# Attention in a fused kernel: where the transposes of the probabilities stand, and how the keys are cut

## What is computed

```python
def _attn_ref(q, k, v):                      # B, H, S, D = 2, 8, 1152, 64
    q_pool = q.reshape(B, H, S // 2, 2, D).mean(axis=3)
    scores = np.matmul(q_pool, k.transpose(0, 1, 3, 2)) / np.sqrt(D)
    scores = scores - np.max(scores, axis=-1, keepdims=True)
    attn = np.exp(scores)
    attn = attn / (np.sum(attn, axis=-1, keepdims=True) + 1e-09)
    return np.matmul(attn, v)

def reference(**kwargs):
    x = _attn_ref(q, k, v).transpose(0, 2, 1, 3).reshape(B * 576, 512)
    x = _moe_ref(x, ...)                     # sigmoid gate, 512 -> 1536 -> 512
    return _moe2_ref(x, ...)                 # 8 experts of width 1024, weights balanced in 8 rounds
```

## Time and profile before

| | us |
|---|---|
| median of 3 runs | 1244.61 (1244.44 to 1244.99) |
| the profiled execution | 1244.73 |
| its span on the core | 1242.9 |
| attention stage, from the start | about 262 |

### The profile page before, as it was taken

The page is one execution under the profiler, slowest core; times in us unless marked ns, Lnnn a source line. Parts: engine busy times, 40 slices in busy tenths (PEclk is TensorE's granted clock), DMA queues, the critical chain, the costliest instruction groups (busy, mean ns, idle before and its releaser), DMA issues.

```text
span 1242.9 us, 19939 instructions
## 1 busy us (share of the span) xinstructions
PE 1232.8 (99%) x7618; PEld 1130.9 (91%) x7618; DVE 798.2 (64%) x1682; ACT 594.6 (48%) x1239; POOL 631.9 (51%) x534
## 2 busy tenths in 40 slices
PE   8999999999999999999999999999999999999999
PEld 7888888899999899999998998998998998998998
DVE  7999999887873144776576376476466466466444
ACT  7999999854433344344353243243243233233221
POOL 6577777737873375654254254254254254254221
PEclk9999999999999999999999999999999999999999
DMA  6677767301112331221221222222222222222112
GB/s 172 120 114 126 120 120 120 87 26 34 52 35 68 111 94 52 68 86 51 69 73 64 69 75 62 68 72 65 67 70 68 68 69 69 64 73 68 52 34 93
DMA packets 98911, 95.37 MB, mean 77 GB/s; under 512 B 14528, under 2 KB 73152, under 8 KB 98816
## 3 DMA queue, kind: packets, MB, share of 16 engines
q1 hardware_dynamic: 98496, 93.77, 30.3%
q10 hardware_dynamic: 320, 0.33, 0.1%
HBM read 88.59 MB, written 2.40 MB: 73 GB/s over the span
## 4 chain that ended last, share of the span: by engine, by line
PE 92%; ACT 5%; DVE 1%; issue 1%; DMA 0%; ACTq 0%; POOL 0%; DVEq 0%; POOLq 0%
PE bank L1253 13%; PE bank L1255 13%; PE bank L1254 13%; PE bank L1506 11%; PE bank L1507 11%; PE bank L1508 11%; PE bank L1138 5%; PE bank L1111 4%; PE bank L1151 3%; PE bank L1152 3%; ACT probs L1615 2%; PE bank L1222 2%; PE bank L1220 2%; PE bank L1221 2%; ACT pT_hi L1534 2%
## 5 line engine op out<-in xcount | busy, mean ns | idle before, releaser
L2201 DVE TENSOR_TENSOR c<-bank,c 128x256 f32<-128x256 f32 (+1 forms) x448 | 197.3, 457 | 281.4 <-PE bank L1255 274.7
L1041 POOL TENSOR_TENSOR w_lo<-w_raw,w_hi 128x512 fp32r<-128x512 f32 x128 | 163.7, 1300 | 287.7 <-ACT w_hi L1534 287.7
L1507 PE MATMUL bank<-w_lo,h_hi 128*128 128x512 f32 x578 | 225.2, 390 | 0.0
L1506 PE MATMUL bank<-w_hi,h_hi 128*128 128x512 f32 x578 | 225.1, 390 | 0.0
L1508 PE MATMUL bank<-w_hi,h_lo 128*128 128x512 f32 x578 | 224.4, 388 | 0.0
L1814 ACT ACTIVATE h_hi<-c 128x256 fp32r<-128x256 f32 (+1 forms) x256 | 112.5, 445 | 160.3 <-DVE c L2201 160.0
L1508 PEld LDWEIGHTS bank<-w_hi,h_lo 128*128 128x128 f32 x578 | 108.5, 188 | 22.9
L1534 ACT ACTIVATE c<-bank 128x256 f32<-128x256 f32 (+1 forms) x64 | 26.2, 410 | 214.7 <-PE bank L1255 214.7
L1506 PEld LDWEIGHTS bank<-w_hi,h_hi 128*128 128x128 f32 x578 | 108.6, 188 | 20.8
L1970 DVE TENSOR_REDUCE part_min<-bank 128x1 f32<-128x256 f32 (+2 forms) x216 | 114.6, 558 | 20.0 <-PE bank L1152 13.7
L1507 PEld LDWEIGHTS bank<-w_lo,h_hi 128*128 128x128 f32 x578 | 108.6, 188 | 20.1
(11 more groups left out here) (206 smaller groups left out, 3142.9 us busy)
## 6 DMA issues: line engine op xcount, KB each, us to landing
w_raw<-in_moe_w SPq DMA_DIRECT2D x64, 512.0 KB, 3.6
w_raw<-in_moe_w SPq DMA_DIRECT2D x64, 256.0 KB, 3.1
q_raw<-in_q SPq DMA_DIRECT2D x30, 288.0 KB, 4.8
k_raw<-in_k SPq DMA_DIRECT2D x30, 288.0 KB, 7.6
wo_raw<-in_moe_w_out SPq DMA_DIRECT2D x16, 384.0 KB, 3.4
v_raw<-in_v SPq DMA_DIRECT2D x16, 288.0 KB, 4.9
gv_raw<-in_moe_w_gate SPq DMA_DIRECT2D x12, 256.0 KB, 2.9
gv_raw<-in_moe_w_val SPq DMA_DIRECT2D x12, 256.0 KB, 3.5
```

The lines of the kernel that those rows point to most:

```text
L1041: ins = nc.gpsimd.tensor_tensor(w2_lo[:, u % 2, c], w2_raw[:, c], f32(w2_hi[:, u % 2, c]), ALU.subtract)
L1506: nc.tensor.matmul(dst, hh, wh, start=(first and c == 0), stop=False)
L1507: nc.tensor.matmul(dst, hh, wl, start=False, stop=False)
L2201: nc.vector.tensor_tensor(dst[:, 0:w], bank[:, (u + b) % 3, 0:w], other[:, 0:w], ALU.add).then_inc(done, 1)
```

## The change

- The keys are cut into three parts of 384 (`KEYS`), at the start of banks 0, 1 and 2. The exponentials take parts 0 and 1 in one instruction of 768 keys, part 2 in one of 384. The pieces in which k is split become 768 and 384 (for the first head 384, 384 and 384).
- The reductions no longer write `part_min`. That of part 0 stores its least in bank 0's last column, next to part 1's first; the reduction of part 1 reads it with its scores and stores the result next to part 2; that of part 2 writes `nmax`. Parts 1 and 2 wait for the reduction before. The small reduction L1972 goes.
- On TensorE the transposes of g-1 stand behind the products with v. Their parts go round a ring of four banks (3, 6, 4, 5), and each waits for the `p_lo` of four parts before.
- ScalarE runs exponentials(g), the copies of outputs, `p_hi`(g-1, 0 to 2), and the splits of k and q. VectorE runs the reductions of g and then `p_lo`(g-2, 0 to 2).
- The common tile has no products with v any more; tiles 5 and 6 have nine instead of six, so that every tile but the common one has nine.

```diff
-KEYS = (0, 256, 640, 1152)
-SCORES_AT = (256, 512, 1024)
-EXP_KEYS = ((0, 640), (640, 1152))
-AV_STEPS = (9, 9, 9, 9, 6, 6, 6, 9, 9)
+KEYS = (0, 384, 768, 1152)
+EXP_PARTS = ((0, 2), (2, 3))
+FILL_RING = (3, 6, 4, 5)
+AV_STEPS = (9, 9, 9, 9, 0, 9, 9, 9, 9)
-KPIECES = ((0, 640), (640, 1152))
-FIRST_KPIECES = ((0, 256), (256, 640), (640, 1152))
+KPIECES = ((0, 768), (768, 1152))
+FIRST_KPIECES = ((0, 384), (384, 768), (768, 1152))
...
         def scores(j):
-            return columns[:, SCORES_AT[j]:SCORES_AT[j] + KEYS[j + 1] - KEYS[j]]
+            return bank[:, j, 0:KEYS[j + 1] - KEYS[j]]
+        def least(j):
+            return columns[:, 512 * j + 511:512 * j + 512]
+        def scores_and_least(j):
+            return columns[:, 512 * j - (j > 0):512 * j + KEYS[j + 1] - KEYS[j]]
         def fill_bank(g, j):
-            if j < 2:
-                return 3 + j
-            return 5 + g % 2 if g < PAIR * NHEAD // 2 - 1 else 5
+            return FILL_RING[(3 * g + j + (g == PAIR * NHEAD // 2 - 1)) % len(FILL_RING)]
...
 (TensorE, tile)
                 score(pair, i, 2)
-                if g >= 1:
-                    for j in range(NKB):
-                        if g >= 2 and j < 2:
-                            pe.wait_ge(p_lo_done, 3 * (g - 2) + j + 1)
-                        fill_p(g - 1, j)
                 if i < COMMON and pair >= 1:
                     ... av(2 * pair - 1, n)
                 if i >= COMMON:
                     ... av(2 * pair, n)
+                if g >= 1:
+                    for j in range(NKB):
+                        freed = 3 * (g - 1) + j - len(FILL_RING) + 1
+                        if freed > 0:
+                            pe.wait_ge(p_lo_done, freed)
+                        fill_p(g - 1, j)
...
 (ScalarE, tile)
-                for n, (k0, k1) in enumerate(EXP_KEYS):
-                    nc.scalar.activation(probs[g % 2][:, k0:k1],
-                                         columns[:, SCORES_AT[2 * n]:SCORES_AT[2 * n] + k1 - k0], ACT.Exp,
+                for n, (j0, j1) in enumerate(EXP_PARTS):
+                    k0, k1 = KEYS[j0], KEYS[j1]
+                    nc.scalar.activation(probs[g % 2][:, k0:k1].rearrange("p (j n) -> p j n", j=j1 - j0),
+                                         bank[:, j0:j1, 0:(k1 - k0) // (j1 - j0)], ACT.Exp,
...
+                outputs(pair, i)
                 if g >= 1:
-                    p_hi(g - 1, 2)
+                    for j in range(NKB):
+                        p_hi(g - 1, j)
                 between(pair, i)
-                p_hi(g, 0)
-                p_hi(g, 1)
...
 (VectorE, tile)
                 for j in range(NKB):
                     dve.wait_ge(s_ready, 3 * g + j + 1)
-                    nc.vector.tensor_reduce(part_min[:, t, j:j + 1], scores(j), AX.X, ALU.min).then_inc(min_done, 1)
-                dve.wait_ge(min_done, 3 * g + 3)
-                nc.vector.tensor_reduce(nmax[:, t:t + 1], part_min[:, t], AX.X, ALU.min).then_inc(nmax_done, 1)
-                if g >= 2:
-                    p_lo(g - 2, 2)
+                    if j >= 1:
+                        dve.wait_ge(min_done, 2 * g + j)
+                    last = j == NKB - 1
+                    nc.vector.tensor_reduce(nmax[:, t:t + 1] if last else least(j), scores_and_least(j), AX.X,
+                                            ALU.min).then_inc(nmax_done if last else min_done, 1)
                 if g < 2:
                     first_q_lo(g + 1)
+                else:
+                    p_lo(g - 2, 0)
+                    p_lo(g - 2, 1)
-                if g >= 1:
-                    p_lo(g - 1, 0)
                 ... reciprocals at i == 1 and i == 8
-                if g >= 1:
-                    p_lo(g - 1, 1)
+                if g >= 2:
+                    p_lo(g - 2, 2)
```

More of the change, by code:

```diff
@@ L164, in build @@
             o_all = allocate(s, [(f"o_all{n}", [PARTS, QLEN], F32) for n in range(ORING)])
-            o_other, r_rows, part_min, nmax, sums, den, rcol, split_scale = allocate(s, [
+            o_other, r_rows, nmax, sums, den, rcol, split_scale = allocate(s, [
                 ("o_other", [PARTS, QLEN], F32),
                 ("r_rows", [PARTS, QLEN], F32),
-                ("part_min", [PARTS, QT, NKB], F32),
                 ("nmax", [PARTS, QT], F32),
@@ L1578, in o_out, with outputs @@
                     copy(o_all[h % ORING][:, cols], bank[:, 7, 0:QHALF]).then_inc(o_copied, 1)
+            def outputs(pair, i):
+                h = 2 * pair
+                if i in (1, 3) and pair >= 1:
+                    o_out(h - 1, 1, i // 2)
+                if i in (6, 8):
+                    o_out(h, 0, i // 2 - 3)
             def between(pair, i):
@@ L1587, in between @@
                     q_hi_part(h + 1)
-                if i in (1, 3) and pair >= 1:
-                    o_out(h - 1, 1, i // 2)
                 if i == 2 and pair == 0:
                     k_hi_part(1, 0)
[L1592 to L1595, removed]
                 if h < LAST:
@@ L1653, in _ @@
             all_tiles(tile)
-            p_hi(PAIR * NHEAD // 2 - 1, 2)
+            for j in range(NKB):
+                p_hi(PAIR * NHEAD // 2 - 1, j)
             o_out(NHEAD - 1, 1, 0)
@@ L2007, in _ @@
             reciprocals(NHEAD - 1, 1)
-            p_lo(g - 2, 2)
+            for j in range(NKB):
+                p_lo(g - 2, j)
             p_lo(g - 1, 0)
```

## The result

The changed kernel takes 1274.65 us (median of six runs, 1274.52 to 1274.88), the kernel before 1244.53 on the same occasion: a ratio of 1.0243, 95% interval 1.023 to 1.0256. It is 2.4% slower, 30.1 us; 1271 us was forecast, in a range of 1256 to 1284.

The account below looks back on a forecast made before the run. TensorE, VectorE and ScalarE stand within 8%, so order decides. A new loop of 3.75 us in 61 plain steps, 4.34 in 8 common ones, plus first steps and entries, makes 271.4 against 245.71 us: 1271 us, range 1256 to 1284.

Parts of the forecast that it names:

- The common tile: Tile common to both heads of a pair, with twelve score products: forecast 4.34 us, against 4.23 before.
- The loop: Every tile: scores, three reductions, two subtractions, third part's transposes, next scores form a closed loop of 3.75 us.
- Term 1: From the start of a tile's scores on TensorE to VectorE's first reduction: 0.63 us.
- Term 2: Three chained reductions on VectorE, up to the start of the first subtraction: 1.66 us.
- Term 3: Two subtractions of 384 columns on VectorE: 1.00 us.
- Term 4: From the wait's end on TensorE through three transposes to the next scores: 0.45 us.
- The signs: Profile after: transposes wait for pT_lo 0.4 to 0.5 us, exponential waits gone, plain step 3.75, common 4.3, pair 34.4 us.
- The end: Behind the last scores: one more tile's stall of 0.4 us, less a narrower last part, in all +0.2.
- Chaining free: Rival: the two chained reduction starts per tile cost what unchained ones do, 14.5 us less, 1256 us; chance 0.12.
- Dear stores: Rival: VectorE's two stores of the least in PSUM cost 0.08 us each, 1282, up to 1293 us; chance 0.15.
- The loop isn't hidden: Denies the rival that the loop closes within TensorE's own 3.23 us, giving a faster 1236 us; chance 0.06.
- Nothing moves: Rival: a loop of some 3.4 us per tile gives the old time; chance 0.03.

Follow-up runs that it names:

- e4: Changed kernel with the transposes put back ahead of the products with v; 1347.32 us, ratio 1.082.
- e5: Changed kernel with the third part's transposes of tile g-1 and their ring wait moved behind tile g+1's first score part; 1268.62 us, ratio 1.0168.
- e6: Changed kernel with the exponentials cut 384 and 768 instead of 768 and 384; 1277.67 us, ratio 1.024.
- e7: Changed kernel with the edits of e5 and e6 together; 1259.02 us, ratio 1.0091.
- e10: e2 with VectorE waiting for all three score parts ahead of the first reduction; 1336.86 us, ratio 1.0724.
- e12: Kernel before with only the equal thirds of keys, the stored least and exponentials of 768 and 384; 1265.33 us, ratio 1.0168.
- e1: Changed kernel with the old least: three unchained reductions into SBUF, then the small reduction; 1262.82 us, ratio 1.0142.
- e2: e1 with reductions 1 and 2 each waiting for the one before; 1287.62 us, ratio 1.0341.
- e3: e1 with the three least values stored in PSUM and read there by the small reduction; 1263.18 us, ratio 1.0144.
- e9: Changed kernel with key parts, exponentials and least as before, third part's transposes of g-1 behind tile g+1's second score part; 1270.68 us, ratio 1.0197.
- e11: e1 with the third part's transposes of tile g-1 moved behind tile g+1's first score part; 1268.80 us, ratio 1.0178.

## Why the prediction was right, point by point

- **The loop** is there as told, by the trace of the changed kernel, by e4, in which the products with v outside the wait's cover cost 1.2 us a step (5.02 against 3.81), and by e5 with e6 and e7, in which taking the ring out makes another limit appear.
- **Term 1**, scores to first reduction: 0.63 forecast, 112.33 - 111.70 = 0.63.
- **Term 2**, reductions to first subtraction: 1.66 forecast, 114.14 - 112.33 = 1.81. This is the term that was mis-sized. The chained starts come 0.10 behind the end instead of 0.035 (113.67 against 112.33 + 1.24 = 113.57): the row they were taken from is of an operation with one wait in front, they have two, as e10 shows. The other 0.02 are reductions of 0.567 instead of 0.558.
- **Term 3**, two subtractions: 1.00 forecast, 1.01.
- **Term 4**, wait's end to next scores: 0.45 forecast, 115.51 - 115.15 = 0.36. Timeline of TensorE in narrow windows, which part the transposes behind the wait:

```profile
115.21 0.33 PE L1117 MATMUL bank<-ident,probs 128*128 128x128 f32 x1
115.38 0.38 PE L1117 MATMUL bank<-ident,probs 128*128 128x128 f32 x2
115.49 0.27 PE L1117 MATMUL bank<-ident,probs 128*128 128x128 f32 x1
```

  TensorE resumes after 0.05; the first transpose then occupies 0.17 instead of 0.11, the second 0.11, and the scores start only 0.03 behind the third. So two things were too large: the resumption costs a transpose 0.06 and not 0.10, and three transposes ahead of scores take some 0.25 and not 0.30 (0.24 in e5, 120.55 to 120.79, where nothing is waited for). On score products the 0.10 does fall, as e12 shows.
- **The step.** Term 2 was 0.15 too short and term 4 0.09 too long. That the forecast of 3.75 is within 0.06 of 3.81 is in part luck: the two errors have opposite signs.
- **The signs.** The transposes wait, but twice in a tile: TensorE's weight loads for them wait 0.46 and 0.16 us (114.74 and 115.21), 0.62 together where 0.4 to 0.5 was told. The waits for exponentials are gone, a pair is 34.74 for 34.4, and the rest is as told.
- **The common tile** takes 4.23 instead of 4.34, by term 4 alone; chaining costs it nothing. The 0.06 at the entry of a head is hidden behind the loop.
- **The sum.** The 71 steps take 281.60 - 6.74 = 274.86 us where 271.4 was forecast: 61 plain ones 0.06 longer, 8 common ones and 15 entries together 1.8 shorter, and the first four, which have waits for the first heads' q and k as well, 4.14, 3.70, 3.93 and 4.20 us. The first scores start 0.63 earlier; that start lies anywhere between 6.5 and 7.5 us in the twelve runs, whatever the edit. The end became 1.4 longer (0.2 was forecast). +29.15 - 0.63 + 1.38 = 29.9, the difference of the spans, 1272.8 - 1242.9. The start's 0.63 is scatter between executions, so it is luck too.
- **The end** was costed too low. VectorE's rows behind the last tile's reductions:

```profile
284.05 1.01 DVE L1917 TENSOR_TENSOR pT_lo<-bank,pT_hi 128x384 fp32r<-128x384 f32 x2
...
285.63 0.52 DVE L1917 TENSOR_TENSOR pT_lo<-bank,pT_hi 128x384 fp32r<-128x384 f32 x1
...
286.30 0.37 PE L1144 MATMUL bank<-pT_hi,v_st 128*128 128x288 f32 x1 [0.64 <-DVE pT_lo L1917]
```

  The third subtraction of tile 69 stands behind an addition and the last denominators, and TensorE's last head waits 0.64 us for it. The prediction priced one tile's stall there and didn't ask who waits for a subtraction that now stands behind these. No run shows what the rest of the 1.4 is.
- **The rivals.** Chaining free is refuted by e1 and e2: three reductions take 1.88 us with waits on each other and 1.49 without, while each signals its semaphore in both. The Trainium skill (page "VectorE: DVE Perf Modes", section "The DRAIN you can't avoid") says, of eight `tensor_copy`, that a semaphore after each operation costs nothing extra; read of a wait on that semaphore, as the prediction read it, this doesn't hold for these reductions. Dear stores in PSUM are refuted by e3. The loop isn't hidden: TensorE's transposes wait in every tile. "Nothing moves" is refuted by the measured time. But a second loop of 3.64 us, through the exponential of 768, was not among the rivals. Had the ring's loop been hidden, the kernel would still have been slower than before, and not 1236 us as that rival said; e5 and e12 show it.

## What to carry to other kernels

When work is moved behind other work on one engine, write down the closed loops, from an operation round through every engine that waits for another back to its successor, and add them up; here, with TensorE busy in 28.71 of 31 us and no engine busier, it was the longest loop and not the busiest engine that set the step. Remove one and ask at once for the next, as two remedies here (e9, e11) failed for want of that: what was put between two score parts delayed the least value, the exponentials and the bank of the next scores. A reduction that waits for its own engine's last result should be priced by a row with as many waits in front of it.

## What the runs showed of the hardware

- Consecutive reductions of VectorE (0.558 us each) start 0.09 us ahead of the end of the one before without a wait on it, 0.03 behind it with that wait alone, 0.10 behind it with two wait instructions (e1, e10, e2). That the second instruction as such is the cause was tested in this one place.
- A store of one value per partition from VectorE to PSUM takes as long as one to SBUF (e3 against e1, 1.50 and 1.49 us for three).
- TensorE resumed behind a wait lost 0.10 us on the first score product (0.28 instead of 0.18 to the next, e12) and 0.06 on the first transpose (0.17 instead of 0.11, changed kernel). Why was not tried.
